# Counting with two columns of levels as the stationary side, routing tiles laid out by expert, and expert weights by plain transfers with a register

## The reference

```
attention: B, H, S, D = 4, 8, 768, 48, a recurrence with complex decay; x = its output as [3072, 384]
# mixture of experts: N = 3072 tokens, E = 8 experts, cap = N // E = 384
logits = x @ w_gate
for idx in np.argsort(-logits.flatten()):          # best pairs (token, expert) first
    tok, e = idx // E, idx % E
    if assigned[tok] >= 0 or counts[e] >= cap: continue
    assigned[tok] = e; counts[e] += 1
for e in range(E):
    out[assigned == e] = relu(x[assigned == e] @ w1[e]) @ w2[e]     # 384 -> 1024 -> 384
out = ((out @ w_a) * (out @ w_b)) @ w_out                           # 384 -> 1536 -> 384
```

## Time and profile before

| | before |
|---|---|
| median of 3 runs | 1211.6 us (1210.97 to 1217.04) |
| the profiled execution | 1213.47 us, of which the span is 1211.4 us |
| TensorE busy | 1094.6 us (90%) |
| VectorE busy | 876.0 us (72%) |
| POOL busy | 591.1 us (49%) |
| ScalarE busy | 513.7 us (42%) |

### The profile page before, as it was taken

The page is one execution under the profiler, slowest core; times in us unless marked ns, Lnnn a source line. Parts: engine busy times, 40 slices in busy tenths (PEclk is TensorE's granted clock), DMA queues, the critical chain, the costliest instruction groups (busy, mean ns, idle before and its releaser), DMA issues.

```text
span 1211.4 us, 37813 instructions
## 1 busy us (share of the span) xinstructions
PE 1094.6 (90%) x14683; PEld 998.3 (82%) x14683; DVE 876.0 (72%) x1881; ACT 513.7 (42%) x961; POOL 591.1 (49%) x583
## 2 busy tenths in 40 slices
PE   2799999999999622999999999999999999999996
PEld 1577777777777522889999999999999999999996
DVE  6889999999899687875775775775775774874221
ACT  6767777777677220313322323323313313313321
POOL 5667777766677225634524524524524524533400
PEclk9899999999999755999999999999999999999998
DMA  6333333333333333022022022021021021021000
GB/s 124 78 70 79 80 83 84 84 84 84 84 84 82 90 117 119 18 71 68 7 72 64 6 78 59 6 80 57 6 83 53 6 84 52 6 86 51 14 7 20
DMA packets 167828, 75.23 MB, mean 62 GB/s; under 512 B 149360, under 2 KB 159344, under 8 KB 167792
## 3 DMA queue, kind: packets, MB, share of 16 engines
q1 hardware_dynamic: 157168, 40.13, 14.9%
q0 software_dynamic: 10624, 34.61, 9.0%
HBM read 65.29 MB, written 9.44 MB: 62 GB/s over the span
## 4 chain that ended last, share of the span: by engine, by line
PE 43%; DVE 14%; issue 4%; ACT 2%; POOL 1%; DMA 0%; DVEq 0%; ACTq 0%; POOLq 0%
PE tb L1870 17%; PE acc L1527 5%; PE acc L1529 5%; PE acc L1528 5%; PE tb L1527 3%; PE tb L1529 2%; PE tb L1528 2%; PE ps_r L1438 2%; DVE slot L1276 2%; DVE ab L1791 1%; ACT ab_high L1700 1%; DVE most L1318 1%; DVE between L1336 1%; POOL w2s L1487 1%; DVE lows L1320 0%
## 5 line engine op out<-in xcount | busy, mean ns | idle before, releaser
L1700 ACT CAST ab_high<-ab 128x384 fp32r<-128x384 f32 x96 | 49.4, 514 | 234.3 <-DVE ab L1791 234.3
L1791 DVE TENSOR_TENSOR ab<-tb,a_sb 128x384 f32<-128x384 f32 x96 | 53.4, 556 | 113.4 <-PE tb L1870 110.7
L1569 POOL TENSOR_TENSOR w_low<-w1s,w_high 128x384 fp32r<-128x384 f32 x62 | 67.2, 1094 | 130.8 <-ACT w_high L1648 130.0
L1575 POOL TENSOR_TENSOR w_low<-w2s,w_high 128x384 fp32r<-128x384 f32 x64 | 79.2, 1237 | 44.5 <-ACT w_high L1657 44.1
L1527 PE MATMUL acc<-wo_high,ab_high 128*128 128x384 f32 x288 | 99.9, 347 | 0.3 <-DVE ab_low L1794 0.3
L1870 PE MATMUL tb<-x_high,wb_high 128*128 128x384 f32 x288 | 98.3, 341 | 0.0
L1529 PE MATMUL acc<-wo_high,ab_low 128*128 128x384 f32 x288 | 97.4, 338 | 0.0
L1870 PE MATMUL tb<-x_high,wa_high 128*128 128x384 f32 x288 | 97.3, 338 | 0.0
L1794 DVE TENSOR_TENSOR ab_low<-ab,ab_high 128x384 fp32r<-128x384 f32 x96 | 53.6, 559 | 60.1 <-ACT ab_high L1700 60.1
L1528 PE MATMUL acc<-wo_low,ab_high 128*128 128x384 f32 x288 | 97.1, 337 | 0.0
L1870 PE MATMUL tb<-x_high,wa_low 128*128 128x384 f32 x288 | 96.4, 335 | 0.0
(11 more groups left out here) (299 smaller groups left out, 3272.0 us busy)
## 6 DMA issues: line engine op xcount, KB each, us to landing
a_re_in<-in_a_re SPq DMA_DIRECT2D x32, 192.0 KB, 3.1
a_im_in<-in_a_im SPq DMA_DIRECT2D x32, 192.0 KB, 3.7
qk<-in_q SPq DMA_DIRECT2D x26, 192.0 KB, 2.7
qk<-in_k SPq DMA_DIRECT2D x26, 192.0 KB, 3.4
vv<-in_v SPq DMA_DIRECT2D x48, 96.0 KB, 2.8
x_rows<-ysb SPq DMA_DIRECT2D x24, 192.0 KB, 2.7
wo_raw<-in_moe_w_out SPq DMA_DIRECT2D x12, 192.0 KB, 2.4
w1s<-in_moe_w_a SPq DMA_DIRECT2D x3, 384.0 KB, 5.0
```

Of the source, the lines that this page charges most:

```text
L1569: nc.gpsimd.tensor_tensor(w1p[1][:, f % NW1, :, :], w1_tile(f), w1p[0][:, f % NW1, :, :].bitcast(F32), ALU.subtract).then_inc(s["w1_low"], 1)
L1575: nc.gpsimd.tensor_tensor(w2p[1][:, f % 2, :], w2s[:, f, :], w2p[0][:, f % 2, :].bitcast(F32), ALU.subtract).then_inc(s["w2_low"], 1)
L1700: nc.scalar.copy(abp[0][:, f % 2, :], ab[:, f % 2, :]).then_inc(s["ab_high"], 1)
L1791: nc.vector.tensor_tensor(ab[:, f % 2, :], tb[(2 * f + 1) % 4][:, 0:CAP], a_sb[:, f % 2, :], ALU.mult).then_inc(s["ab_made"], 1)
```

## The change

- **Counting.** Two neighbouring groups share a matmul: their 2 x 64 levels are the stationary side (128 columns), and their one-hot choices move (2 groups x 8 experts, 16 columns). A round has 12 matmuls. The count of a level is the sum of two blocks of the result: `lacking` is need minus the second, `marks` tells whether the first reaches it. The level is the number of levels that are reached. In the first routing TensorE sums them (`ones` by `marks`), in the others VectorE does it with a reduce, two transposes and four reduces.
- **Layout.** The routing tiles are [128, 8 experts, 24 groups] instead of [128, 24, 8]. Upper bounds are made once after the five rounds. In the first routing several steps drop out, since no token was given before; what only the next routing needs (`keep_given`, `keep_counts`) comes after the token numbers.
- **Weights.** VectorE makes one number, `expert_id`. SP reads it into a register and issues one plain transfer for w1 and one for w2 (`load_expert`). POOL gathers tokens only, straight from `tok_next`.
- **Order.** `ROUTE_LAYERS`, `ROUTE_LAST`, `PIECES_AFTER` and the calls between the `hidden_low` are new. Three pieces of w_a and w_b that VectorE split are POOL's (`MID_LOWS`).

```diff
+FOUND_AT = 64
...
+MID_LOWS = 3
-STEPS = 86
+STEPS = 68
...
-ROUTE_LAYERS = (1, 4, 8, 12)
-ROUTE_LAST = ((0, 0), (2, 0), (3, 0), (4, 1), (7, 1))
+ROUTE_LAYERS = (0, 5, 9, 13)
+ROUTE_LAST = ((1, 0), (3, 0), (4, 0), (5, 0), (7, 0))
...
-PIECES_AFTER = (1, 2, 2, 1, 1, 1, 1, 1)
+PIECES_AFTER = (1, 1, 2, 2, 3, 1, 1, 0)
...
-                    nc.scalar.copy(logits[:, col, :], ps_y[:, 0:E].rearrange("p (o e) -> p o e", o=1)
+                    nc.scalar.copy(logits[:, :, col], ps_y[:, 0:E].rearrange("p (e o) -> p e o", o=1)
...
-        step(v.tensor_tensor(choice[:], same[:].unsqueeze(2).broadcast_to([P, G, QUAD // E, E]),
-                             by_e(free[:]).unsqueeze(2).broadcast_to([P, G, QUAD // E, E]), ALU.mult))
+        step(v.tensor_tensor(choice[:], same[:], to_each_e(free[:]), ALU.mult))
...
             answer()
-            step(v.scalar_tensor_tensor(marks[:], ps_r[one, 0:NTH], need[one, 0:1], iota[one, 0:NTH],
-                                        ALU.is_ge, ALU.mult))
-            step(v.tensor_reduce(highest[one], marks[:], AX.X, ALU.max))
-            step(v.transpose(most_rows[:], highest[one].broadcast_to([QUAD, QUAD])))
-            for q in quads:
-                ins = v.tensor_reduce(everywhere[q], most_rows[:], AX.X, ALU.max)
-            step(ins)
-            step(v.tensor_scalar(lows[:, i + 1:i + 2], everywhere, steps[:, i:i + 1], lows[:, i:i + 1],
+            counted = lambda b: ps_r[b * NTH:(b + 1) * NTH, 0:2 * E].rearrange("p (e b) -> p e b", b=2)[:, :, b]
+            step(v.scalar_tensor_tensor(lacking[of_levels], counted(1), -1.0, need[NTH:P], ALU.mult, ALU.add))
+            level = levels[:, i:i + 1]
+            if alone:
+                v.tensor_tensor(marks[of_levels], counted(0), lacking[of_levels], ALU.is_ge).then_inc(marked, 1)
+                dve.wait_ge(levels_found, i + 1)
+                step(v.tensor_reduce(level, ps_r[:, FOUND_AT:FOUND_AT + E], AX.X, ALU.max))
+            else:
+                step(v.tensor_tensor(marks[of_levels], counted(0), lacking[of_levels], ALU.is_ge))
+                step(v.tensor_reduce(highest[of_levels], marks[of_levels], AX.X, ALU.max))
+                for t in range(0, NTH, QUAD):
+                    ins = v.transpose(level_rows[:, t:t + QUAD], highest[t:t + QUAD].broadcast_to([QUAD, QUAD]))
+                step(ins)
+                for q in quads:
+                    ins = v.tensor_reduce(level[q], level_rows[:], AX.X, ALU.add)
+                step(ins)
+            step(v.tensor_scalar(lows[:, i + 1:i + 2], level, steps[:, i:i + 1], lows[:, i:i + 1],
                                  ALU.mult, ALU.add))
             if i + 1 < NSEARCH:
                 step(thresholds(v, i + 1))
                 yield n[1]
-                compare(v, i + 1, ask, alone)
+                compare(v, i + 1, 0, alone)
                 yield n[1]
-            v.tensor_scalar(over, everywhere, float(NTH - 1), BIG, ALU.is_ge, ALU.mult)
-            step(v.tensor_scalar(above_it, everywhere, 1.0, None, ALU.add))
-            step(v.tensor_scalar(above_it, above_it, steps[:, i:i + 1], lows[:, i:i + 1], ALU.mult, ALU.add))
-            step(v.tensor_scalar(upper[:, i + 1:i + 2], above_it, over, upper[:, i:i + 1], ALU.add, ALU.min))
+                ask(compare(v, i + 1, 1, alone))
...
+        uppers = upper[:, 1:NSEARCH + 1]
+        v.tensor_scalar(over[:], levels[:], float(NTH - 1), BIG, ALU.is_ge, ALU.mult)
+        step(v.scalar_tensor_tensor(uppers, levels[:], 1.0, steps[:], ALU.add, ALU.mult))
+        step(v.tensor_tensor(uppers, uppers, lows[:, 0:NSEARCH], ALU.add))
+        step(v.tensor_tensor(uppers, uppers, over[:], ALU.add))
+        v.tensor_scalar(pos[:, 1, :], best[:], lows[:, NSEARCH:NSEARCH + 1], None, ALU.is_ge)
+        step(v.tensor_reduce(top_edge[:], upper[:], AX.X, ALU.min))
+        step(v.tensor_scalar(pos[:, 0, :], best[:], top_edge[:], None, ALU.is_ge))
+        v.tensor_tensor(sure[:], choice[:], to_each_e(pos[:, 0, :]), ALU.mult)
+        step(v.tensor_tensor(pos[:, 2, :], pos[:, 1, :], pos[:, 0, :], ALU.subtract))
+        step(v.tensor_tensor(between[:], choice[:], to_each_e(pos[:, 2, :]), ALU.mult))
...
+        if alone:
+            step(v.scalar_tensor_tensor(taken[:], behind, float(CAP), between[:], ALU.is_le, ALU.mult))
+        else:
+            step(v.scalar_tensor_tensor(rest[:], ps_r[:, E * G:E * G + E], -1.0, room[:], ALU.mult, ALU.add))
+            step(v.tensor_tensor(taken[:], behind, to_each_g(rest[:]), ALU.is_le))
+            step(v.tensor_tensor(taken[:], taken[:], between[:], ALU.mult))
...
+        step(v.tensor_tensor(count[:], count[:], ps_r[:, 0:E], ALU.add))
+        v.scalar_tensor_tensor(full[:], count[:], float(CAP), waiting[:], ALU.is_ge, ALU.mult)
+        step(v.scalar_tensor_tensor(score[:], count[:], float(CAP), to_emit[:], ALU.is_ge, ALU.mult))
         step(v.tensor_reduce(top[:], score[:], AX.X, ALU.max))
         step(v.scalar_tensor_tensor(chosen[:], score[:], top[:, 0:1], full[:], ALU.is_equal, ALU.mult))
-        v.tensor_tensor(emitted[:], emitted[:], chosen[:], ALU.add)
...
-        for _ in range(NSEARCH):
+        pairs = above.rearrange("p (j b) n -> p j (b n)", b=2)
+        for i in range(NSEARCH):
             first_half()
-            for g in range(G):
-                if alone and g == G // 2:
+            for j in range(G // 2):
+                if alone and j == G // 4:
                     asked()
-                mm = nc.tensor.matmul(ps_r[0:QUAD, 0:NTH], choice[:, g, :, :].rearrange("p r e -> p (r e)"),
-                                      above[:, g, :],
-                                      start=(g == 0), stop=(g == G - 1))
+                mm = nc.tensor.matmul(ps_r[:, 0:2 * E], pairs[:, j, :], choice[:, :, 2 * j:2 * j + 2],
+                                      start=(j == 0), stop=(j == G // 2 - 1))
             mm.then_inc(s["answered"], 1)
+            if alone:
+                pe.wait_ge(marked, i + 1)
+                nc.tensor.matmul(ps_r[:, FOUND_AT:FOUND_AT + E], ones[0:NTH, :], marks[0:NTH, :], start=True, stop=True
+                                 ).then_inc(levels_found, 1)
             yield
...
+    def load_expert(sp, r):
+
+        sp.wait_ge(s["expert_found"], after("expert_found", r, 1))
+        sp.sem_inc(sp_pass, 1)
+        chosen_e = sp.value_load(expert_id[0:1, 0:1], min_val=0, max_val=E - 1)
+        sp.sem_inc(s["expert_taken"], 1)
+        rows_of = lambda w: w[bass.ds(chosen_e, 1), :, :].rearrange("e (k p) n -> p (e k) n", p=P)
+        sp.wait_ge(s["w1_low"], after("w1_low", r, FT1, back=1))
+        sp.dma_start(w1s[:], rows_of(w1)).then_inc(m_sem["w1_gathered"], 16)
+        sp.wait_ge(s["w2_low"], after("w2_low", r, FT1, back=1))
+        sp.dma_start(w2s[:], rows_of(w2)).then_inc(m_sem["w2_gathered"], 16)
...
+            credit(sp, "expert_taken")
+            sp.wait_ge(w_low, EARLY_LOWS)
+            sp.wait_ge(w_high, NPIECE)
+            load_expert(sp, 0)
             for n in range(2):
                 sp.wait_ge(w_low, NRAW - 2 + n + 1)
                 load(NRAW + n, again[n], w_reloaded[n])
+            with sp.Fori(0, E - 1) as p:
+                load_expert(sp, sp.snap(p + 1))
...
-            pool.wait_ge(w_high, NPIECE)
+            pool.wait_ge(w_low, EARLY_LOWS)
             pool.sem_inc(pool_pass, 1)
-            gather_w1(pool, 0)
-            gather_w2(pool, 0, range(1))
             gather_tokens(pool, 0)
-            pool.sem_inc(tokens_sent, 1)
-            gather_w2(pool, 0, range(1, FT1))
+            for i in range(EARLY_LOWS, EARLY_LOWS + MID_LOWS):
+                piece_low(i, homes[i])
...
-            dve.wait_ge(tokens_sent, 1)
             for _ in route_start(dve, 1):
                 pass
-            dve.wait_ge(w_low, EARLY_LOWS)
-            for i in range(EARLY_LOWS, NPIECE - LATE_LOWS):
-                dve.wait_ge(w_high, i + 1)
-                nc.vector.tensor_tensor(piece(i, 1), as_piece(homes[i]), piece(i, 0).bitcast(F32), ALU.subtract
-                                        ).then_inc(w_low, 1)
...
                 hidden_low(p, 0)
+                next(pieces, None)
                 hidden_low(p, 1)
-                next(pieces, None)
-                next(pieces, None)
                 next(pieces, None)
                 hidden_low(p, 2)
                 next(pieces, None)
+                next(pieces, None)
                 hidden_low(p, 3)
-                next(pieces, None)
                 next(pieces, None)
                 hidden_low(p, 4)
                 next(pieces, None)
+                next(pieces, None)
                 hidden_low(p, 5)
-                next(pieces, None)
                 next(pieces, None)
                 hidden_low(p, 6)
                 next(pieces, None)
+                next(pieces, None)
                 hidden_low(p, 7)
-                next(pieces, None)
```

269 lines of the change are left out of this document (124 added, 145 removed).

## The result

The changed kernel took **1196.7 us** (median of 4 runs, 1196.33 to 1199.76) against 1212.9 of the kernel before on the same chip (4 runs): ratio 0.987, 95% interval 0.9835 to 0.990. It is faster, within the range, and 7.9 us above the forecast of 1188.8. The gain is 17 us between the two profiled executions (1213.47 and 1196.34), where 22.8 were forecast.

The account below looks back on a forecast made before the run. The first routing was taken as bound by a VectorE chain, the loop by TensorE. Head 13.5, first expert 4.0 and loop 5.3 sum to 22.8 us off, predicting 1188.8 us from the median; 8-in-10 range 1174 to 1200.

Parts of the forecast that it names:

- The chain through VectorE: First routing: shorter VectorE steps and search rounds make the token numbers ready 11.2 us earlier.
- the gathers of tokens take what they took: Head, after the token numbers: POOL's token gathers keep their pace, 1.27 us from one to the next.
- 0.5 us of delay beside the weights (0 to 3): Head: token gathers share the queues with 3.15 MB of expert weights and lose 0.5 us, bounds 0 and 3.
- 2.5 us for x_low: Head: the first product follows the turned tokens by 2.1 us instead of 4.65, gaining 2.5 us.
- First expert: From the first product to the end of its stretch: earlier w2 and w2_low gain 4.0 us, bounds 1 and 5.
- The counting block: Loop: 12 matmuls replace 24, 0.31 us instead of 0.80, five times, gaining 2.4 us per expert.
- The rival of the stationary load: Counting matmuls: loading 128 columns costs 133 ns each, 1.6 us per block, giving 1234 us; chance 0.04.
- The new wait at hidden_low(7): Loop, before the last layer: TensorE waits 1.65 us per expert, VectorE answering the fourth question first.
- The 0.1s at the two others: Loop, second and third question: 3.3 us of VectorE work against two layers of 3.23, TensorE waiting 0.1 each.
- The 0.5 us for the third compare: Loop, third question: compares slowed while POOL splits weights make TensorE wait 0.5 us per expert.
- No new wait: Rival, loop: no wait at hidden_low(7), so the loop gives 22 us and the total is 1172; chance 0.13.
- Plain transfers late: Rival: the plain w1 and w2 transfers are slow or late, 1190 to 1205 us for a moderate miss; chance 0.06.

Follow-up runs that it names:

- h2: Changed kernel, with SP sending both weights of the first expert only after POOL has issued the three token gathers: 1202.0 us (one run).
- h3: Changed kernel plus one dummy token gather by POOL while the first routing still runs: 1209.8 us (one run).
- h4: h3 with POOL's three weight subtractions behind the token gathers spread over the first expert's first three tiles: 1203.0 us, ratio 0.991 to the kernel before.
- b5: h4 and l357 together, the first expert's w2 sent once POOL has issued the tokens: 1176.3 us, ratio 0.969 to the kernel before.
- b6: b5 with half of the first w2 sent right behind w1, the rest when the third token tile has landed: 1172.1 us, ratio 0.957 to the kernel before.
- h1: Changed kernel, with VectorE standing still from the token numbers until POOL has issued the three token gathers: 1211.7 us (one run).
- l357: Changed kernel with hidden_low(3), (5) and (7) each one routing piece earlier on VectorE: 1179.6 us, ratio 0.9715 to the kernel before.
- c1: l357 with every counting block of the loop issued twice: 1186.0 us, periods 87.8 us.
- l7: Changed kernel with only hidden_low(7) one routing piece earlier on VectorE: 1188.0 us, ratio 0.979 to the kernel before.

## Why the prediction was right, and where it was off

| from the profiled executions | forecast | measured |
|---|---|---|
| token numbers, after VectorE's first `extremes` | 11.2 earlier | 11.0 earlier |
| first product, after `extremes` (the head) | 13.5 earlier | 8.0 earlier |
| start of the routing | same | 1.3 later |
| first expert, product to next turn | 4.75 shorter | 2.65 shorter |
| each of six steady experts | 0.75 shorter | 1.40 shorter |
| last stretch | same | 0.75 longer |
| sum | 22.8 | 17.0 |

(The forecast of the first expert is its 4.0 and one share of the loop.)

- **The chain through VectorE** was right almost to the decimal: a round of 3.91 us where 3.79 was worked out (the threshold step took 0.47 instead of 0.35), numbers ready 38.3 us after the extremes instead of 49.2.
- **The step that failed** is "the gathers of tokens take what they took". I had priced their pace (1.27 us from one to the next, which held at the second and third) and not the start of the first. In the changed kernel POOL begins its first gather 6.4 us after the numbers instead of 1.0. The 5.4 us come once, 2.3 us with nothing in flight (h2), 3.1 more beside the weights, and are off the path altogether when a dummy gather takes them early (h3, h4, b5, b6). That they are a fetch of code is concluded from the packets' times. The kernel before had it in POOL's idle time. No row of before shows the wait, but one thing could have been asked: POOL's next instructions were new ones, behind a wait of 20 us. The Trainium skill ("GPSIMD Engine Reference", Instruction dispatch) has a cost of about 6 us for the first call of POOL code that was loaded at run time, with no instruction in the profile. The 6.4 us are near it, but not the 3.2 to 3.4 without traffic, nor the first indirect transfer of before (1.08 us), and whether it is the same thing no run here shows.
- **0.5 us of delay beside the weights (0 to 3)** should have been the upper end. Where the tokens are issued in time and both weights are in flight, they land after 6.0 us instead of 3.7 (h3, h4); a tile issued beside a starting w2 took 6.8 (b5). In the changed kernel this doesn't show, since POOL is so late that the weights are through: its first tile lands after 3.7 us, before 3.1. Neither end of the range had the right picture. The packets do move in turns (from 467.5 to 470 us of h2, 64 of the gather beside 175 of the weights), but the gather's first packet comes late: 1.7 to 2.3 us after POOL's instruction begins with empty or nearly empty queues (after, h1, b6), 3.3 and 3.4 in h3 and h4, 4.3 for the tile of b5. Why is open. The end of the weights was off as well: 3.15 MB at 348 GB/s from 452 are through at 461, not 463; they were sent at 453.6 and through at 465.5.
- **2.5 us for x_low** came: from the last turned tile to the first product TensorE waits 1.84 instead of 4.65.
- **First expert.** TensorE waited 2.85 us for the last hid_low instead of 1.76, and ran its first 3.9 us at half clock (3.3 before). That is 1.4 of the 2.1 us that are missing; the rest was not traced. The longer wait is again a threshold step, held for 1.42 us by one of POOL's subtractions of w_a and w_b. That POOL's late gather put these there is not shown: with the same order, the first expert takes 86.0 us with the late gather (l357) and 87.4 with the early one (b5), where three of POOL's subtractions lie elsewhere.
- **The counting block** is 0.31 to 0.32 us as forecast, and c1 shows that most of the time counts. The rival of the stationary load is dead: 26 ns per matmul, not 107 or 133.
- **The new wait at hidden_low(7)** is there: 1.76 us where 1.65 was worked out, in each expert, and l7 shows that the order makes it (1.5 us of 1.76 come back). The 0.1s at the two others are 0.16 and 0.19.
- **The 0.5 us for the third compare** did not come, and that is most of why the loop gave 1.4 and not 0.75. VectorE's waits for TensorE's answers (0.93 at the third question) had room for it. What the forecast lacked here was not a mean but a coin: the slowing by POOL was known from the earlier trace rows for compares of 1.8 us, and taken as a smooth 0.5; it falls on the 0.31 us threshold step as all or nothing, 0 or 0.8 us of TensorE's time, twice per expert. In the profiled execution it fell on one of twelve; with all twelve the loop would have given nothing (90.5).
- **The rivals.** "No new wait" would have given 1172 by the forecast; made to come true by l357 it gave 1179.6, most of the difference (5.5 us) being the head. "Plain transfers late" pointed at the right place for the wrong reason: w1 landed at 460.7, in time; it was the gathers that were late. The register read is within its cover: from the expert's number to SP's transfer it took 1.2 us.
- **Luck.** The head gave 5.5 us less than forecast and the loop 3.9 more; that the total is near owes something to these errors having opposite signs, and something to how few threshold steps were held.
- Unexplained: the start of the routing (1.3 us later; it varies by 6 us between executions) and 0.75 us in the last stretch. Neither was tested.

## What to carry to other kernels

Price the start of a chain's next engine as well as its pace: an engine that goes on to new code behind a long wait may have to fetch it on the path, and slower beside the transfers that a change has just made early; a dummy of the same kind in its idle time takes that off. Send only those bytes ahead of a small urgent transfer that are needed first. And where a VectorE chain feeds TensorE beside POOL's copies, order it so that the step TensorE waits for comes first; an order that holds by hundredths of a microsecond is kept in one expert and lost in the next.

## What the runs showed of the hardware

- POOL's first gather behind its long wait begins 3.2 to 3.4 us after what it waits for without traffic, 6.4 to 6.8 beside 3.15 MB of plain transfers, against 1.0 us later on. A packet of an instruction queue moves 2.0 to 2.4 us ahead of it; that this is POOL's code is concluded.
- Token gathers of 0.2 MB land 3.0 to 3.7 us after issue with no plain transfer in flight, and 4.4 to 7.1 us after it when 1.5 to 3 MB of plain transfers are under way or start (h2, h3, b5). The plain transfers move some 360 GB/s (2.9 MB from 456 to 464 us); 3.15 MB, issued at 453.6 and 454.1, had landed at 465.5.
- The threshold step (0.31 us, on SBUF) ends with POOL's subtraction if it begins up to 0.10 us ahead of it or behind it by the profile, and is not held if it begins earlier (96 meetings). A step of 0.36 us was held for 5.7 us by three subtractions in a row, another in h1 for 7.2 us by five, with no gap used between them.
- A matmul with 128 bf16 columns of stationary side and 16 moving columns costs 26 ns in a row of twelve or 24.
